# First units of a banded attention: three score products in their own PSUM banks, earlier distances, reordered first loads

## The reference

```python
scores = scale * np.matmul(q, k.transpose(0, 1, 3, 2))
is_global = pos[None, :] < int(n_global)            # n_global = 8
is_local = (rel >= 0) & (rel < int(n_local))        # n_local = 96
dist = np.where(is_global & ~is_local, float(n_local), np.abs(rel))
bias = -slopes[:, None, None] * dist
scores = np.where(is_global | is_local, scores + bias, -1e9)
a = softmax(scores);  x = a @ v                     # heads side by side: (2, 768, 512)
# moe: u = x + (x^T U V)^T;  x = u + relu(u @ w_ch1) @ w_ch2      # 512 -> 2048 -> 512
# moe2: xk, xr = mixes of x and x shifted by one position
#       out = sigmoid(xr @ w_r) * (relu(xk @ w_k)**2 @ w_v)
```

## Time and profile before

| what | us |
|---|---|
| three timed executions | 516.47, 517.46, 519.26; median 517.46 |
| the profiled execution, its own time | 519.25 |
| its span, first to last instruction | 517.4 |
| PE busy in the span | 500.2 (97%) |
| DVE, ACT, POOL busy | 184.1, 130.5, 242.8 |
| granted TensorE clock, mean | 0.999 |

### The profile page before, as it was taken

The page is one execution under the profiler, slowest core; times in us unless marked ns, Lnnn a source line. Parts: engine busy times, 40 slices in busy tenths (PEclk is TensorE's granted clock), DMA queues, the critical chain, the costliest instruction groups (busy, mean ns, idle before and its releaser), DMA issues.

```text
span 517.4 us, 9414 instructions
## 1 busy us (share of the span) xinstructions
PE 500.2 (97%) x3664; PEld 412.4 (80%) x3664; DVE 184.1 (36%) x480; ACT 130.5 (25%) x352; POOL 242.8 (47%) x234
## 2 busy tenths in 40 slices
PE   3989999999999999999999999999999999999997
PEld 2778787778888888888888888888888888888885
DVE  6777774131322313222131231311443233441223
ACT  3887884111001010010110101121322132212220
POOL 4055675173009000099500829980999579960000
PEclk9999999999999999999999999999999999999999
DMA  6987775004002200024400000000000200020002
GB/s 207 301 270 236 241 240 187 1 5 159 0 1 81 81 0 0 0 82 162 162 0 0 1 0 1 0 0 0 1 0 1 82 0 0 0 81 0 0 0 81
DMA packets 15343, 34.48 MB, mean 67 GB/s; under 512 B 1488, under 2 KB 1872, under 8 KB 15312
## 3 DMA queue, kind: packets, MB, share of 16 engines
q1 hardware_dynamic: 14736, 33.14, 19.0%
q10 hardware_dynamic: 576, 0.92, 0.6%
HBM read 30.91 MB, written 3.15 MB: 66 GB/s over the span
## 4 chain that ended last, share of the span: by engine, by line
PE 96%; DVE 2%; issue 1%; DVEq 0%
PE psum L590 25%; PE psum L578 25%; PE psum L643 13%; PE psum L634 13%; PE psum L658 6%; PE psum L429 4%; PE psum L467 3%; PE psum L443 2%; PE psum L459 1%; PE psum L475 1%; PE psum L482 1%; DVE probs L872 1%; PE psum L490 1%; DVE reach L827 0%; DVE result L1028 0%
## 5 line engine op out<-in xcount | busy, mean ns | idle before, releaser
L980 DVE SCALAR_TENSOR_TENSOR HL<-psum,HH 128x512 fp32r<-128x512 f32 x48 | 33.2, 692 | 173.3 <-ACT HH L770 173.3
L770 ACT ACTIVATE HH<-psum 128x512 fp32r<-128x512 f32 x48 | 28.8, 600 | 230.4 <-PE psum L578 230.4
L578 PE MATMUL psum<-UH,w1l 128*128 (+1 forms) x192 | 74.8, 390 | 0.6 <-issue 0.6
L590 PE MATMUL psum<-HH,w2h 128*128 128x512 f32 x192 | 75.1, 391 | 0.0
L578 PE MATMUL psum<-UH,w1h 128*128 (+1 forms) x192 | 74.8, 390 | 0.0
L590 PE MATMUL psum<-HH,w2l 128*128 128x512 f32 x192 | 74.7, 389 | 0.0
L590 PE MATMUL psum<-HL,w2h 128*128 128x512 f32 x192 | 74.7, 389 | 0.0
L578 PE MATMUL psum<-UL,w1h 128*128 (+1 forms) x192 | 74.7, 389 | 0.0
L1110 POOL TENSOR_SCALAR w1h<-raw 128x2048 fp32r<-128x2048 f32 x4 | 7.7, 1917 | 118.2 <-PE psum L590 118.2
L1018 DVE TENSOR_TENSOR k_square<-k_relu 128x512 f32<-128x512 f32 x24 | 24.2, 1010 | 66.3 <-ACT k_relu L795 66.2
L689 ACT ACTIVATE probs<-probs,neg_max 128x192 f32<-128x192 f32 x96 | 42.5, 444 | 15.8 <-DVE neg_max L872 14.8
(11 more groups left out here) (111 smaller groups left out, 856.8 us busy)
## 6 DMA issues: line engine op xcount, KB each, us to landing
v_in<-in_v SPq DMA_DIRECT2D x16, 384.0 KB, 4.7
raw<-in_moe_w_ch SPq DMA_DIRECT2D x6, 1024.0 KB, 5.2
k_in<-in_k SPq DMA_DIRECT2D x7, 512.0 KB, 5.5
v_rest<-in_v_rest SPq DMA_DIRECT2D x8, 384.0 KB, 4.2
out<-result SPq DMA_DIRECT2D x12, 256.0 KB, 2.0
q_in<-in_q SPq DMA_DIRECT2D x7, 384.0 KB, 3.7
raw<-in_moe_w_ch SPq DMA_DIRECT2D x8, 256.0 KB, 4.5
raw<-in_moe_w_v SPq DMA_DIRECT2D x2, 1024.0 KB, 5.1
```

Of the source, the lines that this page charges most:

```text
L578: mm = pe.matmul(bank[4 + f % 2][:, 0:BLK], w[:, kt, f * P:(f + 1) * P], x[:, kt, ds(blk * BLK, BLK)], start=kt == 0 and n == 0, stop=kt = ...
L590: mm = pe.matmul(bank[d][:, 0:BLK], w[:, f, d * P:(d + 1) * P], x[:, f % 2, :], start=f == 0 and n == 0, stop=f == FQ - 1 and n == 2)
L770: act.activation(HH[:, f % 2, :], bank[4 + f % 2][:, 0:BLK], ACT.Relu).then_inc(hid_high, 1)
L980: dve.scalar_tensor_tensor(out=HL[:, f % 2, :], in0=bank[4 + f % 2][:, 0:BLK], scalar=0.0, in1=HH[:, f % 2, :].bitcast(F32), op0=ALU.max, ...
```

## The change

1. PE first runs nine 128x128 products of zeros (`WARM_UPS`, `zeros`, a corner of `probs` that DVE clears first) into bank 6. Then scores(0), scores(1) and scores(2) are issued one behind another, each into two banks of its own: (0, 1), (4, 5), (6, 7). scores(3) then waits only for the maxima of units 0 and 1 (unit 1 has its banks), later ones as before. `banded_attention` on PE begins at n = 2 with turn(0).
2. ACT issues the loads of q and k of pair 1 behind those of pair 0, and scales both parts of pair 0's q with two activations. POOL no longer does that; it computes `glob_far` in place of DVE.
3. DVE builds the band part in place in the second half of `reach`; `grid` is gone. Three memsets, four copies and one later memset replace four memsets and six copies; the cast of the counts moves up between them.
4. `more_distances` copies the windows of tile 2 before those of tile 3, and maxima(1) waits for each apart (`dist_more` at 5 and 9).
5. SP issues pair 0's v as soon as pair 0's q and k have landed, with no wait for scores, then, once pair 1's q and k have landed, U, V and mu; it waits for pair 0's v before it goes on to pair 2.
6. Pieces of the first weight quarter follow pairs 2, 3, 4 (two), 5 and 6 in place of pairs 1 to 6. POOL splits them in the same places.

```diff
+        FIRST_SCORE_BANKS = [(0, 1), SCORE_BANKS, (6, 7)]
+        def score_bank(n, h):
+            return bank[(FIRST_SCORE_BANKS[n] if n < UNITS else SCORE_BANKS)[h]]
+        WARM_UPS = 9
+        zeros = probs[:, 1, 1, 2 * WIN - P:2 * WIN]
...
+            quarters = {2: (0,), 3: (1,), 4: (2, 3), 5: (4,), 6: (5,)}
             sp.dma_start(counts_i[:, :], counts.partition_broadcast(P)).then_inc(counts_in, 16)
             sp.wait_ge(qk_in[0], 32)
-            for p in range(PAIRS):
+            load_rest(0)
+            load_main(0, 0)
+            load_main(0, 1)
+            sp.wait_ge(qk_in[1], 32)
+            sp.dma_start(U[:, :, :], mix_u).then_inc(uv_in, 16)
+            sp.dma_start(V4[:, :], mix_v).then_inc(uv_in, 16)
+            sp.dma_start(mu[:, :, :], mus).then_inc(mu_in, 16)
+            sp.wait_ge(v_landed[0], 48)
+            for p in range(1, PAIRS):
+                sp.wait_ge(qk_done, UNITS * p)
...
-                if n >= 1:
+                if n == UNITS:
+                    pe.wait_ge(max_done, 2 * n - 2)
+                elif n > UNITS:
                     pe.wait_ge(max_done, 2 * n)
...
-                for n in range(1, NU + 3):
-                    if 2 <= n < NU + 2:
+                scores(1)
+                scores(2)
+                for n in range(2, NU + 3):
+                    if n < NU + 2:
                         turn(n - 2)
...
-                    if n < NU:
+                    if UNITS <= n < NU:
                         scores(n)
...
+            pe.wait_ge(zeros_set, 1)
+            for _ in range(WARM_UPS):
+                pe.matmul(bank[MIX_BANKS[0]][:, 0:P], zeros, zeros, start=True, stop=True)
             scores(0)
...
+            act.dma_start(q_in[:, 1, :], qt[1]).then_inc(qk_in[1], 16)
+            act.dma_start(k_in[:, 1, :], kt_[1]).then_inc(qk_in[1], 16)
             act.wait_ge(counts_step, 1)
             act.activation(warm_up[:, :], counts_f[:, 0:1], ACT.Exp, scale=0.0)
+            act.wait_ge(scale_set, 2 * PPB)
+            for landed, cols in ((first_in, slice(0, FIRST)), (qk_in[0], slice(FIRST, S))):
+                act.wait_ge(landed, 32)
+                act.activation(q_in[:, 0, cols], q_in[:, 0, cols], ACT.Copy, scale=q_scale[:, 0:1]).then_inc(q_scaled, 1)
...
-                if n == 1:
-                    dve.wait_ge(dist_more, 9)
...
+                        if n == 1 and h == 0:
+                            dve.wait_ge(dist_more, 5 + 4 * i)
...
+            pool.tensor_scalar(glob_far[:, :], key[:, :], counts_f[:, 2:3], FAR, ALU.is_ge, ALU.mult).then_inc(glob_step, 1)
+            pool.wait_ge(glob_step, 1)
+            pool.tensor_scalar(glob_far[:, :], glob_far[:, :], counts_f[:, 0:1], 0.0, ALU.max, ALU.add).then_inc(glob_step, 1)
             pool.wait_ge(scale_set, 2 * PPB)
-            pool.wait_ge(first_in, 32)
-            prepare_q(0, slice(0, FIRST))
-            pool.wait_ge(qk_in[0], 32)
-            prepare_q(0, slice(FIRST, S))
...
-                    if 1 <= p < PAIRS - 2:
-                        split_piece(p - 1)
-                    if p == PAIRS - 3:
-                        split_piece(p)
+                    for k in {2: (0,), 3: (1,), 4: (2, 3), 5: (4, 5)}.get(p, ()):
+                        split_piece(k)
```

More of the change, by code:

```diff
@@ L397, in _ @@
                 load_main(p, 1)
[L398 to L403, removed]
+                for k in quarters.get(p, ()):
+                    load_piece(k)
             for c in range(2, NCH):
@@ L808, in reaches @@
             def reaches():
+                one = reach[:, WIN:2 * WIN]
+                span = one[:, GLOB:WIN]
                 dve.wait_ge(reach_step, GROUPS)
                 dve.wait_ge(grids, 1)
-                dve.tensor_scalar(grid[:, :], grid[:, :], group_base[:, 0:1], None, ALU.subtract).then_inc(reach_step, 1)
+                dve.tensor_scalar(span, span, group_base[:, 0:1], None, ALU.subtract).then_inc(reach_step, 1)
                 dve.wait_ge(reach_step, GROUPS + 1)
-                dve.tensor_scalar(behind[:, :], grid[:, :], 0.0, FAR, ALU.is_lt, ALU.mult).then_inc(reach_step, 1)
@@ L816, in reaches @@
-                dve.wait_ge(reach_step, GROUPS + 2)
-                dve.tensor_tensor(grid[:, :], grid[:, :], behind[:, :], ALU.max).then_inc(reach_step, 1)
-                dve.wait_ge(grids, 3)
-                for g, a, z in ((0, GLOB, GLOB + P), (1, 0, GROUP), (2, GROUP, GROUP + GLOB), (3, 0, GLOB)):
-                    at = g // 2 * WIN
-                    dve.memset(reach[group(g % 2), at + a:at + z], FAR).then_inc(reach_step, 1)
-                dve.wait_ge(reach_step, GROUPS + 3)
-                for g, a, z, s in ((0, GLOB + P, WIN, P), (1, GROUP, P, GROUP), (1, P + GLOB, WIN, P), (2, 0, GROUP, 0),
-                                   (2, GROUP + GLOB, WIN, GROUP), (3, GLOB, WIN, 0)):
-                    at = g // 2 * WIN
-                    dve.tensor_copy(reach[group(g % 2), at + a:at + z],
-                                    grid[group(g % 2), s:s + z - a]).then_inc(reach_step, 1)
+                dve.tensor_scalar(behind[:, :], span, 0.0, FAR, ALU.is_lt, ALU.mult).then_inc(reach_step, 1)
@@ new lines, in reaches @@
+                dve.wait_ge(grids, 3)
+                dve.memset(reach[group(0), GLOB:P + GLOB], FAR).then_inc(reach_step, 1)
+                dve.memset(reach[group(1), 0:GROUP], FAR).then_inc(reach_step, 1)
+                dve.memset(one[group(1), 0:GLOB], FAR).then_inc(reach_step, 1)
+                dve.wait_ge(reach_step, GROUPS + 2)
+                dve.tensor_tensor(span, span, behind[:, :], ALU.max).then_inc(reach_step, 1)
+                dve.wait_ge(counts_in, 16)
+                dve.tensor_copy(counts_f[:, :], counts_i[:, :]).then_inc(counts_step, 1)
@@ new lines, in reaches @@
+                dve.wait_ge(reach_step, GROUPS + 6)
+                dve.tensor_copy(one[group(0), 0:GLOB], one[group(0), GLOB:2 * GLOB]).then_inc(reach_step, 1)
+                dve.tensor_copy(reach[:, P + GLOB:WIN], one[:, P + GLOB:WIN]).then_inc(reach_step, 1)
+                dve.tensor_copy(reach[group(1), GROUP:P], one[group(1), GROUP + GLOB:P + GLOB]).then_inc(reach_step, 1)
+                dve.wait_ge(reach_step, GROUPS + 7)
+                dve.tensor_copy(one[group(0), GLOB:2 * GLOB], one[group(0), 2 * GLOB:3 * GLOB]).then_inc(reach_step, 1)
@@ L830, in _ @@
+                dve.wait_ge(reach_step, GROUPS + 10)
+                dve.memset(one[group(0), GROUP:GROUP + GLOB], FAR).then_inc(reach_step, 1)
+            dve.memset(zeros, 0.0).then_inc(zeros_set, 1)
             for j in range(PPB):
```

44 lines of the change are left out of this document (19 added, 25 removed).

## The result

| | us |
|---|---|
| changed kernel, 4 runs | 521.99 to 524.33, median **523.75** |
| kernel before, 4 runs | 516.47 to 519.26, median 517.17 |
| ratio of changed to before, 95% interval | 1.010 (1.007 to 1.013) |
| profiled execution after: its own time, span | 523.73, 521.7 |
| the same of before | 519.25, 517.4 |

The change makes the kernel slower, by some 1%. The forecast was 514.0 with a range up to 516.2. The span grew by 4.3 us.

What follows compares the result with a forecast made beforehand. PE was taken to bound the running attention and everything from 85 us, so only the start could gain. Unit 4's first exponential, 3.5 us sooner with other terms at zero, turned a median of 517.46 into 514.0; range 511.9 to 516.2.

Steps and rivals of the forecast that it cites:

- What bounds the kernel: PE is nearly always busy in the running attention and from 85 us; only time gained before the pipeline fills counts.
- Distances: DVE's work at the start: 0.85 us shorter (0.4 to 1.2), first maxima at 7.6 instead of 8.46.
- q on ACT: ACT's scaling of pair 0's q: 0.45 us, second part 0.5 to 0.9; scores(0) at 5.6, at most 6.0.
- ACT as the pacer up to exps(4): Early attention units: ACT paces at 2.32 us each, exps(4) at 17.15 instead of 20.65, a gain of 3.5 us.
- at the high level 0.55 + 0.85: Before exps(3): PE's turn(1) and scores(3) take 0.55 and 0.85 us at the high clock, ready at 14.5, in time.
- the clock falls back: Rival, chance 0.10: PE's clock is low in units 3 and 4, 0.8 us more each; gain 1.9, time 515.6.
- Loads, weight pieces: Attention loads: reordered transfers cause no wait, bound 1.3 us; moved first-quarter weight pieces are worth zero.
- I take no wait: Loads for the early pairs: pair 2's q is scaled by 18.5 for scores(6) at 20.1; no wait, bound 1.3 us.
- the transfers are late: Rival, chance 0.12: pair 1's v or pair 2's q comes 1.3 us late; gain 2.2, time 515.3.
- Products of zeros: PE's start: nine products end at 5 to 5.8 us; any delay of scores(0), up to 0.3, is covered by distances.
- gaps in PE's issue: Rival, chance 0.04: more late-instruction stops among PE's matmuls, 2.1 us each of the longest kind; with three, 520.3.
- The first large product 3.5 us sooner: Sign in the next profile, at the attention's end: the large products start 3.5 us sooner.

Runs made afterwards that it cites:

- e4: Changed kernel without the nine products of zeros: 515.53 us, 0.997 of the kernel before.
- e3: Changed kernel with the nine products of zeros in a hardware loop instead of written out: 515.46 us, 0.996 of the kernel before.
- e5: Changed kernel with the zeros in a loop, plus a loop of ten more products on PE behind turn(0): 517.26 us, 0.998 of the kernel before.
- e12: Changed kernel without zeros, with the weight pieces behind pairs 1 to 6 as before: 515.34 us, 0.999 of the kernel before.
- e9: Changed kernel without zeros, with SP's 1 MB chunk loads held until the first large products are done: 513.34 us, 0.994 of the kernel before.
- e6: Changed kernel, zeros still written out, with SP's 1 MB chunk loads held until the first large products are done: 516.95 us, 0.998 of the kernel before.
- e11: Kernel before with nine never-run products in PE's dense branch, and SP's 1 MB chunk loads held: 518.49 us, 1.005 of the kernel before.
- e7: Kernel before with four products added to PE's dense branch, which never runs: 519.97 us, 1.003 of the kernel before.
- e2: Kernel before with nine products added to PE's dense branch, which never runs: 521.96 us, 1.010 of the kernel before.
- e1: Changed kernel without the mixing loop of PE's dense branch, which never runs: 517.14 us, 0.998 of the kernel before.
- e10: Kernel before with SP's 1 MB chunk loads held until the first large products are done: 516.76 us, 1.000 of the kernel before.

## Where the prediction was right and wrong

- **What bounds the kernel:** right, as far as data and engines go. PE is busy behind 20 us. That "what starts them sooner moves the end by the same amount" failed: exps(4) came 1.25 sooner, the end of the attention 0.95, and the large products later, since PE waited for its instructions.
- **Distances:** first maxima at 7.20 for 7.6; the gain was 1.26, a little above the upper bound of 1.2. **q on ACT:** 0.49 and 0.72, inside the bounds; scores(0) at 5.60 as forecast. POOL's nine copies were done at 9.93 (9.75) and exps(1) came at 10.37 (10.2). These steps held.
- **ACT as the pacer up to exps(4): mis-sized.** The term "at the high level 0.55 + 0.85" for turn(1) and scores(3) failed in the changed kernel: 0.90 and 1.56. The step itself was right, as e4's 17.05 shows. This is the rival "the clock falls back", which forecast a gain of 1.9; it was 1.25 in this trace. I took the unbroken work from 1.3 to 10.5 as the reason against it; the level fell in PE's idle 2.5 us behind it (0.75 from 10.2 to 12.7). In the medians of e3 and e4 the start is worth 2.2 us, where I wrote 3.5. That the Trainium skill (TensorE: Matmul & The Clock Gate, Part 4: PE-mode transpose) sets transposes apart is neither confirmed nor refuted by these runs: e5 put ordinary products beside them and its level stayed up, but so did e4's without.
- **Loads, weight pieces:** right for the data. In the changed kernel's trace no row of PE in the attention waits for a load, and e12 is level with e4. But the step "I take no wait" held only as long as the start was late: in e4, whose exps(4) came at 17.05, PE stands for 0.67 us at 21.60 ahead of the first weigh_rest of pair 1, whose v landed at 21.5. The rival "the transfers are late" was thus true there, by less than its 1.3. POOL scaled pair 2's q at 19.75 and not by 18.5, and nothing waited for it. What the estimate left out is that PE's own code comes through the same transfers.
- **Products of zeros: this step failed.** They were costed at their run time alone, at zero, since they end "still under the cover of the distances". They did, at 5.14. But every instruction written out also moves all code behind it, and I never asked what lies behind a jump. Their price was 8.2 us by the medians (523.75 - 515.53), the whole difference between faster and slower; without them the time lies inside the forecast range. In the traces four to five of these 8.2 us are the stop behind the jump and the clock behind it.
- **The rival "gaps in PE's issue":** the right resource, for the wrong reason and with a wrong price. I read the four gaps as chance, in proportion to the load on the DMA engines, priced them at 2.1 each and wanted three. There were six in place of four, but the five in the attention add up to 3.1 for 3.5 before. What cost was one, of 4.0, at a fixed place, and with 2.0 behind it for the clock. "The load per pair doesn't grow" didn't bear on it. The rows that would have told were there: counted in matmuls, the four stops of the earlier trace rows lie at 4.7, 8.7, 10.7 and 14.0 times 125.4 records: one grid for the first three, and the last, behind the jump, off it.
- **"The first large product 3.5 us sooner":** it came 3.07 later. The last sign that I named was a start of the large products that moves by 3.5 and a time that doesn't follow. It didn't come like that: the start itself moved the wrong way, and the time followed.

## What to carry to other kernels

Count the instructions that a change writes out, not only their run time: where a long program jumps over a branch that isn't taken, place the target well ahead of a block's edge or keep large transfers away from the jump (513.34 in e9), and put repeated filler in a loop. If a kernel moves by some us for no reason in its data flow, look for rows "<-issue", count the matmuls up to them, look whether an instruction packet ended 1 to 2 us ahead, and add or remove code that never runs. Price a warm-up with the time that it holds others back: here nine products of zeros gained nothing (e3 and e4), and ten more that kept the level up gained nothing either (e5).

## What the runs showed of the hardware

- PE's instructions arrive in blocks of 16 KB (0.34 MB in 21 packets), about 125.4 matmuls with their weight loads. At some of their edges PE stands for 0.2 to 2.1 us in the attention, while transfers are busy, and goes on 1.2 to 1.6 us after a packet has ended. The Trainium skill (Runtime: NRT & Kernel Launch, Instruction fetch mechanics) gives the same size, 256 instructions, and says that a branch to a place outside what is loaded makes the engine wait; with both the traces agree (125.4 matmul records, and the stops of 0.95 and 1.78 at the jump of e6 and e11). It also calls the crossing of an edge mostly hidden; here it wasn't: up to 2.09.
- The packet with the block behind the jump started as a 1 MB load ended (ten traces), and 0.8 to 1.5 us before the attention's end where the load was held (four). Where the load was issued 3.0 to 3.4 us ahead of the jump, PE got the block 3.8 to 4.1 us behind it (eight traces); without the load, 0.95 (e6) and 1.78 us (e11).
- Code that never runs made the kernel before slower by 2.3 (e7) and 4.3 us (e2).
- 4 us of idle cost another 2.0: the clock was granted at 0.50 for ten products. It also fell behind idle of 1.85 (e1) and 2.32 us (e2) inside the attention and of 2.69 at the jump (e7); idle of 2.09 (before, at 39.00), 2.23 (e5), 1.78 (e11), 1.42 (e2) and 0.95 us (e6) left it at 1.00. The length of one idle stretch doesn't decide it.
- The kernel before scatters from 514.8 to 524.0 over 31 runs. Its traces and those of its variants show gaps of different size at like places (2.09 and 0.91 before; 1.56 and 1.19 in e10). That these make the scatter is likely but was not tested.
- Open: why the clock level at 12 to 18 us differs between executions of like code, why v was slow in e2, and what the 8.2 us are made of beyond the jump.
